# Capacity-limited routing with 16-bit pair comparisons, one-hot rows on VectorE, 128-column weights, and idle products in the first two searches

## The reference

```python
# attention: scores only between rows of the same cluster; output x is (1536, 512)
def _moe_ref(x, w_gate, w1, w2):
    N, D = x.shape
    E = w_gate.shape[1]            # 8
    cap = N // E                   # 192
    flat = (x @ w_gate).flatten()
    order = np.argsort(-flat)
    assigned = -np.ones(N, dtype=np.int64)
    counts = np.zeros(E, dtype=np.int64)
    for idx in order:
        tok, e = (int(idx) // E, int(idx) % E)
        if assigned[tok] >= 0 or counts[e] >= cap:
            continue
        assigned[tok] = e
        counts[e] += 1
        ...
    for e in range(E):
        mask = assigned == e
        out[mask] = np.maximum(x[mask] @ w1[e], 0.0) @ w2[e]
# second mixture: out += p[:, e] * (relu(x @ v1[e]) @ v2[e]) for 4 experts
```

## Time and profile before

| | us |
|---|---|
| median of 3 runs (lowest, highest) | 1056.09 (1056.0, 1059.53) |
| the profiled execution | 1053.91 |
| its span, first to last instruction | 1052.1 |
| PE busy | 1011.7 (96%) |
| DVE, ACT, POOL busy | 617.7, 485.3, 438.8 |

### The profile page before, as it was taken

The page is one execution under the profiler, slowest core; times in us unless marked ns, Lnnn a source line. Parts: engine busy times, 40 slices in busy tenths (PEclk is TensorE's granted clock), DMA queues, the critical chain, the costliest instruction groups (busy, mean ns, idle before and its releaser), DMA issues.

```text
span 1052.1 us, 17855 instructions
## 1 busy us (share of the span) xinstructions
PE 1011.7 (96%) x6392; PEld 927.4 (88%) x6392; DVE 617.7 (59%) x1306; ACT 485.3 (46%) x953; POOL 438.8 (42%) x359
## 2 busy tenths in 40 slices
PE   5999999999977999999999999999999999999996
PEld 4889999999966999999998999988999988899995
DVE  5788888888866555552405555444578544555542
ACT  4788888888810333336332332332353232233320
POOL 5043332324001111111466865655647855665542
PEclk9999999999975999999999999999999999999999
DMA  4233323332155657569932122212212412221201
GB/s 116 69 80 80 88 76 91 80 80 57 30 122 126 155 171 178 175 171 275 182 95 81 41 81 80 62 59 81 73 49 80 141 43 79 80 60 61 81 1 60
DMA packets 87744, 99.60 MB, mean 95 GB/s; under 512 B 18560, under 2 KB 57472, under 8 KB 87680
## 3 DMA queue, kind: packets, MB, share of 16 engines
q1 hardware_dynamic: 84976, 92.40, 32.2%
q0 software_dynamic: 2704, 6.33, 2.1%
HBM read 79.81 MB, written 6.32 MB: 82 GB/s over the span
## 4 chain that ended last, share of the span: by engine, by line
PE 91%; DVE 4%; ACT 2%; DMA 1%; POOL 1%; issue 1%; SPq 0%; DVEq 0%; ACTq 0%; POOLq 0%
PE ps_y L1452 9%; PE ps_y L1453 9%; PE ps_y L1451 9%; PE ps_h L1478 8%; PE ps_y L1493 8%; PE ps_h L1453 6%; PE ps_h L1451 6%; PE ps_h L1452 6%; PE ps_t L1356 6%; PE ps_s L1343 4%; PE ps_o L1370 3%; PE ps_o L1371 3%; PE ps_s L1344 3%; PE ps_m L1317 2%; PE ps_m L1390 2%; PE ps_y L1555 2%
## 5 line engine op out<-in xcount | busy, mean ns | idle before, releaser
L577 POOL TENSOR_TENSOR w_lo<-w_sum,w_hi 128x1792 fp32r<-128x1792 f32 x32 | 129.8, 4080 | 62.3 <-ACT w_hi L795 62.3
L1453 PE MATMUL ps_y<-b_lo,h_hi 128*128 128x512 f32 x384 | 149.7, 390 | 0.0
L1452 PE MATMUL ps_y<-b_hi,h_lo 128*128 128x512 f32 x384 | 149.7, 390 | 0.0
L1451 PE MATMUL ps_y<-b_hi,h_hi 128*128 128x512 f32 x384 | 149.4, 389 | 0.0
L1270 DVE SCALAR_TENSOR_TENSOR Y<-ps_y,mix_n,Y 128x512 f32<-128x512 f32 x84 | 63.0, 750 | 134.9 <-PE ps_y L1453 134.9
L1451 PE MATMUL ps_h<-x_hi,w_hi 128*128 128x384 f32 x384 | 128.6, 335 | 0.0
L1453 PE MATMUL ps_h<-x_lo,w_hi 128*128 128x384 f32 x384 | 128.5, 335 | 0.0
L1452 PE MATMUL ps_h<-x_hi,w_lo 128*128 128x384 f32 x384 | 128.4, 334 | 0.0
L583 POOL TENSOR_TENSOR b_lo<-b_raw,b_hi 128x2048 fp32r<-128x2048 f32 x16 | 74.0, 4627 | 115.9 <-ACT b_hi L802 115.9
L1001 DVE TENSOR_TENSOR p_lo<-ps_t,p_hi 128x384 fp32r<-128x384 f32 x192 | 99.9, 548 | 29.0 <-ACT p_hi L725 27.5
L992 DVE TENSOR_REDUCE neg_max<-ps_s 128x1 f32<-128x768 f32 x96 | 91.2, 950 | 17.0 <-PE ps_s L1344 17.0
(11 more groups left out here) (203 smaller groups left out, 2290.3 us busy)
## 6 DMA issues: line engine op xcount, KB each, us to landing
w_sum<-in_moe_w_dram SPq DMA_DIRECT2D x64, 256.0 KB, 3.2
b_raw<-in_moe_w_dram SPq DMA_DIRECT2D x16, 1024.0 KB, 5.2
raw_a<-in_moe_w_dram SPq DMA_DIRECT2D x8, 1024.0 KB, 9.6
raw_b<-in_moe_w_dram SPq DMA_DIRECT2D x8, 1024.0 KB, 13.3
odd_a<-in_moe_w_dram SPq DMA_DIRECT2D x8, 1024.0 KB, 9.2
odd_b<-in_moe_w_dram SPq DMA_DIRECT2D x8, 1024.0 KB, 15.3
khhT<-kqT SPq DMA_DIRECT2D x32, 192.0 KB, 2.9
raw_k<-in_k_dram SPq DMA_DIRECT2D x16, 192.0 KB, 2.4
```

The source lines that it names most:

```text
L577: g.tensor_tensor(w_lo[t][:], w_sum[t][:, 1:8], w_hi[t][:].bitcast(F32), ALU.subtract).then_inc(wlo_done[t], 1)
L1451: t_.matmul(dst, w_hi, x_hi, start=first, stop=False)
L1452: t_.matmul(dst, w_lo, x_hi, start=False, stop=False)
L1453: return t_.matmul(dst, w_hi, x_lo, start=False, stop=last)
```

## The change

- `reach` is compared from 16-bit inputs that lie in pairs: `level`, `steps`, `cur` and `slot` become bf16, the last two hold every value twice, and digit 0 gets a copy `dig_0` of its own. Before the first comparison DVE now waits for all its earlier steps, `cand` among them. `token_ids(n - 1)` stands ahead of the first comparison in every phase.
- `slot_hot` is made by DVE for every expert (`slots_hot`), right behind `slot` and ahead of `pen` and the next phase. ACT's two steps, `slot_far` and the semaphore `far_step` are gone. `slot_hot` has 32 more columns at its end, set to zero.
- The counts use 128 weight columns for 6-bit digits too (the rest of `reach` is old data, and the rows it makes aren't read), and so does `slot_tokens`.
- `slot_tokens(n - 1)` stands ahead of digit 0's count in every phase. `gathered_rows(0)` stands ahead of digit 2's count of the second phase. The tables are new, with idle products between count and spread as well, and 40 ahead of the first `slot_tokens`. In the second phase the first real product stands before digit 3's count.
- At the end `slot_tokens(6)` stands ahead of `slot_ranks(7)`.

```diff
--- before.py
+++ after.py
@@ -52,14 +52,14 @@
-    F_FIRST = (0,) * 7 + (2, 5, 2, 6, 4)
-    F_SECOND = (14, 2, 0, 2, 5, 2, 6, 2, 6, 2, 6, 4)
-    F_PHASE = (16, 2, 0, 2, 5, 2, 6, 2, 6, 2, 8, 2)
-    F_TOKENS = [0, 0, 8] + [11] * (E - 4)
+    F_FIRST = (0,) * 6 + (3, 1, 3, 1, 5, 0)
+    F_SECOND = (14, 2, 10, 2, 9, 2, 9, 2, 9, 2, 11, 0)
+    F_PHASE = (12, 2, 7, 2, 6, 2, 6, 2, 6, 2, 9, 0)
+    F_TOKENS = [0, 0, 8] + [8] * (E - 4)
     FILLS = [(0,) * 12, F_FIRST, F_SECOND] + [F_PHASE] * (E - 4)
-    WARM = [(30, 0, 18, 0, 12, 0, 12, 0, 12, 0, 16, 0), (14, 0, 18, 0, 12, 0, 12, 0, 0, 0, 0, 0)]
+    WARM = [(58, 7, 23, 7, 16, 7, 16, 7, 16, 4, 30, 0), (48, 7, 23, 7, 3, 7, 0, 0, 0, 0, 0, 0)]
     WARM += [(0,) * 12] * (E - 3)
-    H_SPLIT = [2] + [5] * (E - 3)
+    W_TOKENS = [0, 40] + [0] * (E - 3)
     assert B == 2 and D == 64 and 2 * D == P and TPB == 6 and E == 8 and C == 16 and KD == 4 and KF == 4
@@ -90,9 +90,9 @@
         ones_t = sb("ones_t", [P, 2 * NT], F32)
-        steps = sb("steps", [P, CAP], F32)
+        steps = sb("steps", [P, CAP], BF16)
         steps_k = sb("steps_k", [P, KMAX], F32)
-        level = sb("level", [P, ND, KMAX], F32)
+        level = sb("level", [P, ND, KMAX], BF16)
         unit = sb("unit", [P, ND - 1, NT], F32)
@@ -167,8 +167,7 @@
         rows_in = sb("rows_in", [P, 2, DM], F32)
-        slot_hot = sb("slot_hot", [P, NT, CAP], BF16)
-        slot_far = sb("slot_far", [P, NT, CAP], BF16)
+        slot_hot = sb("slot_hot", [P, NT * CAP + P - CAP // 2], BF16)
         h1 = sb("h1", [P, 2 * KF, CAP], F32)
@@ -183,7 +182,8 @@
         dig = sb("dig", [P, ND - 1, NT], F32)
-        cur = sb("cur", [P, 2, NT], F32)
+        cur = sb("cur", [P, 2, NT, 2], BF16)
+        dig_0 = sb("dig_0", [P, NT, 2], BF16)
         same = sb("same", [P, NT], F32)
@@ -198,7 +198,7 @@
         rank = sb("rank", [P, 2, NT], F32)
-        slot = sb("slot", [P, 2, NT], F32)
+        slot = sb("slot", [P, 2, NT, 2], BF16)
         pen = sb("pen", [P, NT], F32)
...
@@ -504,6 +503,7 @@
                                     ALU.add).then_inc(levels_in, 1)
+                g.memset(slot_hot[:, NT * CAP:], 0.0).then_inc(levels_in, 1)
@@ -825,18 +825,6 @@
-            def slot_far_tiles(n, tiles):
-                act.wait_ge(slot_ready, n + 1)
-                at_least(act, hot_ready, n)
-                for t in tiles:
-                    s.activation(slot_far[:, t, :], steps[:], ACT.Abs, bias=slot[:, n % 2, t:t + 1],
-                                 scale=-1.0).then_inc(far_step, 1)
-
-            def slot_hot_tiles(n):
-                act.wait_ge(far_step, NT * n)
-                at_least(act, ids_full, n)
-                s.activation(slot_hot[:], slot_far[:], ACT.Relu, bias=ones_t[:, 0:1], scale=-1.0).then_inc(hot_ready, 1)
-
             def rows_1(m):
...
@@ -865,17 +845,10 @@
             for n in range(E - 2):
-                if n > 0:
-                    between_tiles(n, range(H_SPLIT[n - 1], 2 * KF))
-                    slot_hot_tiles(n)
                 results_and_rows(n)
-                for j in range(H_SPLIT[n]):
+                for j in range(2 * KF):
                     hidden_1(n, j)
...
-            between_tiles(E - 2, range(H_SPLIT[E - 3], 2 * KF))
-            slot_hot_tiles(E - 2)
-            slot_far_tiles(E - 1, range(NT))
-            slot_hot_tiles(E - 1)
             results_and_rows(E - 2)
...
@@ -1096,17 +1069,21 @@
                 dve.wait_ge(rank_full, n + 1)
-                at_least(dve, far_step, NT * (n - 2))
                 link(v_.scalar_tensor_tensor(out=rank[:].rearrange("p a t -> p (a t)"), in0=ps_rt[:, 16:16 + 2 * NT],
...
                                              op0=ALU.add, op1=ALU.mult))
-                v_.tensor_tensor(slot[:, n % 2, :], rank[:, 0, :], rank[:, 1, :], ALU.add).then_inc(slot_ready, 1)
-
-            def first_slots_hot():
-
-                hot = [P, NT, CAP]
-                v_.tensor_tensor(slot_hot[:], spread(steps[:], 1, hot), spread(slot[:, 0, :], 2, hot),
-                                 ALU.is_equal).then_inc(hot_ready, 1)
+                pair = [P, NT, 2]
+                v_.tensor_tensor(slot[:, n % 2], spread(rank[:, 0, :], 2, pair), spread(rank[:, 1, :], 2, pair),
+                                 ALU.add).then_inc(slot_ready, 1)
+
+            def slots_hot(n):
+
+                hot = [P, NT, CAP // 2, 2]
+                dve.wait_ge(slot_ready, n + 1)
+                at_least(dve, ids_full, n)
+                v_.tensor_tensor(slot_hot[:, 0:NT * CAP].rearrange("p (t c two) -> p t c two", t=NT, two=2),
+                                 spread(steps[:].rearrange("p (c two) -> p c two", two=2), 1, hot),
+                                 spread(slot[:, n % 2], 2, hot), ALU.is_equal).then_inc(hot_ready, 1)
@@ -1128,16 +1105,20 @@
                 link(v_.tensor_reduce(pick[:], m2[:], AX.X, ALU.max))
+                add(v_.tensor_copy(dig_0[:], spread(dig_i[:, 0, :], 2, [P, NT, 2])))
                 add(v_.tensor_tensor(cand[:], m2[:], spread(pick[:], 2, shape), ALU.is_equal))
...
-                if n == 1:
-                    token_ids(0)
+                if n > 0:
+                    token_ids(n - 1)
+                dve.wait_ge(r_step, r_count[0])
...
                     K = 1 << bits
-                    now = dig_i[:, 0, :] if i == 0 else cur[:, i % 2, :]
-                    ks = [P, NT, K]
-                    v_.tensor_tensor(reach[:, :, 0:K], spread(now, 2, ks), spread(level[:, i, 0:K], 1, ks),
+                    now = dig_0[:] if i == 0 else cur[:, i % 2]
+                    ks = [P, NT, K // 2, 2]
+                    v_.tensor_tensor(reach[:, :, 0:K].rearrange("p t (k two) -> p t k two", two=2),
+                                     spread(now, 2, ks),
+                                     spread(level[:, i, 0:K].rearrange("p (k two) -> p k two", two=2), 1, ks),
                                      ALU.is_ge).then_inc(reach_ready, 1)
@@ -1146,16 +1127,15 @@
                         link(v_.tensor_tensor(dig[:], dig_i[:, 1:ND, :], unit[:], ALU.mult))
-                    if i == 1 and n > 1:
-                        token_ids(n - 1)
                     dve.wait_ge(cnt_full, ND * n + i + 1)
...
                         dve.wait_ge(digit_full, ND * n + i + 1)
-                        link(v_.scalar_tensor_tensor(out=cur[:, (i + 1) % 2, :], in0=now, scalar=ps_rt[:, 0:1],
-                                                     in1=dig[:, i, :], op0=ALU.subtract, op1=ALU.add))
+                        link(v_.scalar_tensor_tensor(out=cur[:, (i + 1) % 2], in0=now, scalar=ps_rt[:, 0:1],
+                                                     in1=spread(dig[:, i, :], 2, [P, NT, 2]), op0=ALU.subtract,
+                                                     op1=ALU.add))
                     else:
...
@@ -1179,10 +1159,8 @@
                 take_slots(n)
-                dve.wait_ge(slot_ready, n + 1)
-                if n == 0:
-                    first_slots_hot()
-                link(v_.tensor_scalar(pen[:], slot[:, n % 2, :], 0.0, GONE, ALU.is_lt, ALU.mult))
+                slots_hot(n)
+                link(v_.tensor_scalar(pen[:], slot[:, n % 2, :, 0], 0.0, GONE, ALU.is_lt, ALU.mult))
                 link(v_.tensor_tensor(logit[:], logit[:], spread(pen[:], 2, shape), ALU.add))
@@ -1197,6 +1175,7 @@
             token_ids(E - 2)
+            slots_hot(E - 1)
             token_ids(E - 1)
@@ -1502,8 +1481,6 @@
                     m, st = k // (2 * S_E), k % (2 * S_E)
-                    if k == 0:
-                        gathered_rows(0)
                     if st < S_E:
@@ -1527,7 +1504,8 @@
                     for t in range(NT):
-                        mm = t_.matmul(ps_tok[0:HS, 2 * s:2 * s + 2], slot_hot[:, t, s * HS:(s + 1) * HS],
+                        c = t * CAP + s * HS
+                        mm = t_.matmul(ps_tok[:, 2 * s:2 * s + 2], slot_hot[:, c:c + P],
                                        place[:, t, :], start=(t == 0), stop=(t == NT - 1))
@@ -1542,20 +1520,21 @@
                     K = 1 << bits
-                    if n == 1 and i == 0:
-                        keep_running(20)
-                        slot_tokens(0)
-                    if n > 1 and i == 1:
+                    if n > 0 and i == 0:
                         products(F_TOKENS[n])
+                        keep_running(W_TOKENS[n])
                         slot_tokens(n - 1)
...
                     keep_running(warm[2 * i])
+                    if n == 1 and i == 2:
+                        gathered_rows(0)
                     pe.wait_ge(reach_ready, ND * n + i + 1)
                     for t in range(NT):
-                        mm = t_.matmul(ps_cnt[0:K, 0:E], reach[:, t, 0:K], cand[:, t, :], start=(t == 0),
+                        mm = t_.matmul(ps_cnt[:, 0:E], reach[:, t, :], cand[:, t, :], start=(t == 0),
                                        stop=(t == NT - 1))
...
                     products(fill[2 * i + 1])
```

(11 more changed lines are left out.)

13 lines of the change are left out of this document (3 added, 10 removed).

## The result

The changed kernel takes 1038.81 us (median of 4 runs, 1038.4 to 1039.53); the kernel before took 1056.05 us beside it (1054.27 to 1059.53, 4 runs). The ratio is 0.9834, with a 95% interval of 0.9808 to 0.9859: faster by 1.7%. The forecast was 1040.7 us with a range of 1034 to 1049. The profiled execution has a span of 1036.7 us (before 1052.1) at a mean granted clock of 0.994 (before 0.979). The medians are 17.2 us apart and the two profiled executions 15.4: the profiled execution before was 2.1 us faster than its median, the one after 0.35. MoE in what follows is a mixture of experts; the second MoE is the second mixture. A chunk is the 192 tokens of one expert, numbered by the phase that closes it.

What follows compares the result with a forecast made beforehand. Bounds: latency of the first two searches until PE has expert 0's rows, then PE's instruction times in program order. 11.2 + 3.1 + 4.8 - 2.7 - 0.7 - 0.3 = 15.4 us saved; median 1040.7 us, range 1034 to 1049.

Steps and rivals of the forecast that it cites:

- Part 1: VectorE comparisons: 16-bit pairs halve the slope, 1.76 to 0.96 us (7-bit), 0.96 to 0.56 (6-bit), `slot_hot` 2.56 to 1.36.
- rival B: VectorE comparisons: pairs run at the single rate, only 5.3 us of gain left, 1050.8 us; chance 0.08.
- Part 2: TensorE weight loads: 128 columns save 3.1 us over seven `slot_tokens` and 4.8 us over fifteen 6-bit counts.
- Part 3: First two searches: expert 0's rows reach PE earlier, despite a 1.4 us wait; `slot_ranks(1)` near 334.9, 11.2 us gained.
- Part 4: Idle products in both first searches: price 0, clock holds except an even chance of falling at the rows, 0.7 us lost.
- Part 5: `slot_hot` on VectorE: no new wait, 0.6 us to spare at the tightest; 0.3 us allowed for expert 0's late `raw_b`.
- Part 6: End of routing: PE idles 3.9 us instead of 1.8 for expert 6's rows, plus 0.6 us half clock; 2.7 us lost.
- Rival A: End of routing: the last rows land as quickly as elsewhere, no idle or cold stretch, 1034.5 us; chance 0.14.
- D: Gathers of experts 2 to 5 compete with weights and land late, 1052 to 1066 us; chance 0.11.
- E: TensorE wide loads pay by width, costing 9.5 us instead of gaining 7.9, 1062.7 us; chance 0.01.

Runs made afterwards that it cites:

- ids first: Changed kernel with token_ids(6) ahead of take_slots(7) on VectorE, so expert 6's ids no longer wait for the last ranks: 1038.78 us, ratio 0.9855.

## Why the prediction was right, point by point

The sum came out at 15.4 us, and 15.4 us were measured between the spans. That is better than its terms deserve, and the exact hit is luck: the first searches brought 1.2 us less than the sum had and the columns 0.8 less, the end cost 1.3 us less and `raw_b` 0.3 less, and the attention, which nothing changed, ended 0.34 us earlier. The median came out at 1038.8 instead of 1040.7, because the profiled executions stand at different distances from their medians.

- Part 1 (pairs): right in each of the three durations. The run without them gives 1051.1 us; rival B, the same case, had been priced at 1050.8, though with other shares than it had: 0.20 to 0.86 us of waiting for the tokens, mostly 0.47, where it said 0.65, less in the first two (3.0 instead of 6.8, since the wait for the rows gave way), more at the end (6.1, where it had none).
- Part 2 (columns): 0.45 us for a token block was measured at 0.46. For a 6-bit count I took the upper end, 0.32, and it was 0.17 on PE's queue, the lower end, with another 0.1 from the products around it. A steady search takes 25.87 us, not 25.7. Over the searches that is 0.8 us too much in the sum.
- Part 3 (first searches): predicted 11.2 us less 0.7 for the clock, measured 9.3 (45.91 - 35.92 = 10.0, less two products' 0.66). The steps of the search went as written; the rows did not. I took the distance from `ids` to the landing from the earlier trace rows, 6.1 us; now the gathers took 4.2 and 4.7 us to land instead of 4.0 and 3.1, and it was 7.0. The wait in front of them became 2.4 instead of 1.4 us. The rest, some 0.5 us, is the clock.
- Part 4 (idle products): their price was 0 but for the place in front of the rows, where a fall was given an even chance, and it came. It cost about 1.3 us, not 1.5: with fp32 pairs there was no fall, and from rows to ranks(1) it took 8.93 us with three comparisons that are 0.4 us slower each. Elsewhere the clock held, with PE busy 96% and not 90%. What the idle products bring was no term of its own in the sum; it is small, at most 1.3 us by the rows.
- Part 5 (one-hot rows on VectorE): no new wait in the steady searches, as worked out. The run without pairs shows how near it was: with 2.56 us instead of 1.36 the token block waits in every one.
- Part 6 (the end): right in kind, a wait of 3.2 us where 3.9 were expected and 1.8 stood before, with the half clock costing as much as before: 1.4 us lost and not 2.7. Two steps of it missed in opposite directions: the landing was taken for 7.4 us and was 7.0 and 6.3, and the gathers were taken to be issued 1.3 us apart and were 2.2, because the first stood beside the one-hot rows that the change itself puts on VectorE. Part 5, which found no new wait from that move, had not looked at GpSimd. Part 5's 0.3 for a late `raw_b` was not paid at all.
- Behind `slot_ranks(1)` the sum expected 7.9 - 2.7 - 0.3 = 4.9 us and got 201.49 - 196.40 + 0.66 = 5.75. With the 9.3 ahead of it and an attention that ended 0.34 us earlier in this execution that is 15.4.
- One sentence of the sum was wrong without harm here: that GpSimd's chain to the second MoE "hangs on the same gathered rows as PE, so it moves with PE". The run with the ids first moved PE by 3.3 us and that chain by 1.2; had the end gained more than it did, that sentence would have cost 2.5 us. Rival A (no wait at the last rows, 1034.5 us) rested on it too: the wait alone taken away gave 1038.8, and 1034.5 was measured only when the queue on ScalarE was put in order as well. That this is rival A's figure is luck: its price for the wait and the cold stretch was 6.2 us, and the end gained 4.1.
- Rivals D and E fell: the gathers of experts 2 to 5 landed after 3.1 to 4.5 us and PE never waited for them, expert 1's after 6.4 to 7.0 with time to spare; and wide loads are faster, not slower.

## What to carry to other kernels

A change of several parts can be priced part by part when each is on the engine that sets the time in its stage: here three prices summed, within the noise, to what all three cost together. Its order of work can be a loss by itself and right only for the faster parts; who takes over such an order without them gets the loss. And a wait that is removed near the end of a stage is won only when the next queue is looked through as well: which engine holds, behind an operand that comes from elsewhere, work that TensorE wants soon.

## What was not expected of the hardware

- Two bf16 inputs that are each spread (stride 0) along one axis, with pairs kept side by side on the last, run a comparison at the double rate: 0.96 us for 1536 elements, 1.36 for 2304, against 1.76 and 2.56 in fp32.
- Half clock for 30.7 us cost some 1.3 us at most, since PE was busy for 11.8 of them and none of the long waits was for PE. After holes of 1.3 to 2.4 us in front of the rows the clock was at half for 3.4 us in some executions, for 6.8 and 13.7 in others; no run separates what sets that length.
- The same pair of 96-row gathers landed after 3.1 us at the shortest and 13.2 at the longest within one kernel; with 4 MB of weights held back beside it (two layers' loads) it landed some 2.5 us sooner.
- A gather's instruction on GpSimd that starts while VectorE compares runs until some 0.9 us after the comparison's end: 1.88 us beside 1.36 us of one-hot rows, 3.08 us beside 2.56, and 0.99 with none beside it.
